# Two rows of TensorE products against one row interleaved by threes

## The chip, the cores and the metric

The kernel runs on one core of one Trainium2 chip. The metric is device time in microseconds (us), the median of several executions; lower is better.

## The reference

A linear attention layer feeds a dense two-layer network, and that feeds eight experts, of which each token takes one. All sizes are fixed: 2 x 768 = 1536 tokens, model width 384, dense width 2048, expert width 1024.

```
# attention: B, H, S, D = 2, 8, 768, 48
cur = k_t (outer) v_t * u ;  y_t = r_t @ (state + cur) ;  state = w * state + k_t (outer) v_t
# dense network on the 1536 x 384 result (the part that the change touches)
h = x @ w_in                                   # 384 -> 2048: "first layer"
g = np.where(h > 0.0, h, np.exp(np.minimum(h, 0.0)) - 1.0)
x2 = g @ w_out                                 # 2048 -> 384: "second layer"
# experts: argmax of x2 @ w_gate picks one of 8, at most 384 tokens each
h = np.maximum(np.einsum('ecd,edf->ecf', disp, w1), 0.0)
y = np.einsum('ecf,efd->ecd', h, w2)           # scaled by the gate and put back in token order
```

## The kernel before

Every float32 product is made of three faster products on values split in a high and a low half (`hi`, `lo`): hi x hi, hi x lo, lo x hi. The helper `product` issues these three matmuls, and so their lines in the profile are always L1362, L1363 and L1364, whatever they compute; the tile names tell them apart. `bank<-xt,wd_hi` with 256 moving columns is the first layer of the dense network, `bank<-wd_hi,g_hi` (or `g_lo`) with 392 moving columns the second (384 columns of x2 and 8 router logits).

The dense network runs over NB = 6 blocks n of 256 tokens, and in each over FT = 16 steps f of 128 hidden units; q = 16 n + f numbers the steps. In step q TensorE (PE) issues, in program order:

- `fc1(n, f)`: nine matmuls of the first layer (three slices of the model width, three matmuls each) into PSUM bank `ps_h[f % 2]`. The last one raises the semaphore `s_h`. Before the first, PE waits for `s_g` >= q - 1, that is, until the bank has been read for step q - 2.
- in some steps products of the attention (`scores`, `back`, `outer`), of the routing (`count`, `logits`) or transposes;
- `fc2` of three steps earlier (LAG = 3): six matmuls, three for each of the two tiles of 128 tokens, into `ps_x2[0]` and `ps_x2[1]`. Before the first, PE waits for `s_glo` of step q - 3. Sixteen such steps accumulate into one pair of banks. The last of a block (in step f = 2 of the next block) raises `s_fc2`; the first of the next block (in step f = LAG = 3) waits until both banks have been copied out (`s_x2`).

Between the two layers lies the function g, on four engines in a row for each step: VectorE (DVE) takes the minimum with 0 (L1182, which waits for `s_h`), ScalarE (ACT) the exponential (L866), VectorE the maximum (L1190, raises `s_g`), ScalarE rounds to the high half (L875, `s_ghi`), GpSimd (POOL) subtracts to get the low half (L707, `s_glo`). `elu` has two buffers, `g_hi` and `g_lo` have four. Each of these engines works its own list in order, and other work is written into that list behind the step's own part:

- VectorE: copying x2 out of its bank (L1155, in step f = 2 after L1190), and the router: `shift`, `choose`, `gates` and `place_rows` in steps 7, 8, 9 and 11 of block 1, in steps 3, 6, 7 and 9 of blocks 2 to 4, and in steps 3, 5, 6 and 9 of block 5; in block 5, from step 5 on, also the low halves of the first expert's weights (L1165), between L1182 and L1190.
- ScalarE: the other copy of x2 (L834), and in block 5 in every second step a cast of the first expert's weights (L856).
- GpSimd: keys, queries, decay and diagonals of the attention, and the scatter of routed rows (L683).

The order is written by hand; nothing is scheduled by a planner. A table (`PLANS`, read by `chunk_for`) says in which step a piece of the attention is due. `route(n)` is the same for the router.

Of the kernel before, what the change touches and what calls it, by code (L numbers as in the profile page):

```python
# [12 lines left out]
def build(nc, B, H, S, D, DFF, NE, FE, CAP, rkt_in, nat_in, decay, bonus, bonus_pair, win, wout, wouttr, wgate, wexp, out, slots):  # L13
    T = B * S
    C = 128
# [4 lines left out]
    KT = DM // 128  # L20
    BT = 2
    BN = BT * C
    NB = T // BN
    FT = DFF // 128
# [15 lines left out]
    LAG = 3  # L40
# [38 lines left out]
    def new(name, shape, dtype=F32):  # L79
        return put(name, shape, dtype)[0]  # L80
# [32 lines left out]
    wd_hi = new("wd_hi", [128, WI + FT * WO], F32R)  # L113
    wd_at = top[0]
    wd_lo = new("wd_lo", [128, WI + FT * WO], F32R)
# [8 lines left out]
    xt = [new(f"xt{b}", [128, KT, 2, BN], F32R) for b in range(2)]  # L124
    pwk2 = put("pwk2", [128, HP, C], F32, top[0])[0]
    g_hi = new("g_hi", [128, 4, BN], F32R)
    prod = put("prod", [128, 2, HP, C], F32, top[0])[0]
    g_lo = new("g_lo", [128, 4, BN], F32R)
# [48 lines left out]
    with ctx:  # L177
        bank = [ctx.enter_context(nc.psum_tensor(f"bank{i}", [128, 512], F32)) for i in range(8)]

        ps_h, ps_x2, ps_s, ps_y = bank[0:2], bank[2:4], bank[4:6], bank[6:8]  # L180
# [7 lines left out]
        def sem(name):  # L188
            return ctx.enter_context(nc.semaphore(name))
# [54 lines left out]
        s_h = sem("h_done")  # L244
        s_m = sem("min_ready")
        s_exp = sem("exp_ready")
        s_g = sem("g_ready")
        s_ghi = sem("g_hi_ready")
        s_glo = sem("g_lo_ready")
        s_fc2 = sem("fc2_done")  # L250
# [65 lines left out]
        F_T, F_LG = 3, 6  # L316
        F_WG, F_WGT = 12, 14

        def route(n):

            return dict(zip(("shift", "choose", "gates", "count", "place", "scatter"),
                            (7, 8, 9, 10, 11, 11) if n == 0 else
                            (3, 6, 7, 8, 9, 12) if n < NB - 2 else (3, 5, 6, 8, 9, 10)))
        F_W1 = 2
        F_X = 5
        F_A, F_E0 = 9, 5
# [33 lines left out]
        def chunk_for(what, n, f):  # L360

            for c, steps in PLANS.items():
                if steps.get(what) == FT * n + f:
                    return c
            return None
# [21 lines left out]
        def leaves_state(c):  # L387
            return c % PER != PER - 1
# [13 lines left out]
        def wait_if(eng, s, count):  # L402

            if not (isinstance(count, int) and count <= 0):
                eng.wait_ge(s, count)
# [4 lines left out]
        def w_in_cols(f, kt):  # L410

            return slice((f * KT + kt) * 128, (f * KT + kt + 1) * 128)
# [5 lines left out]
        def gated_cols(f):  # L418

            return slice(WI + f * WO, WI + (f + 1) * WO)  # L420

        def x2_cols(n):

            return slice(NE if n == 0 else 0, WO)
# [932 lines left out]
        def _(pe):  # L1357
            mm = nc.tensor.matmul

            def product(dst, w_hi, w_lo, x_hi, x_lo, start, stop):  # L1360

                mm(dst, w_hi, x_hi, start=start, stop=False)  # L1362
                mm(dst, w_hi, x_lo, start=False, stop=False)  # L1363
                return mm(dst, w_lo, x_hi, start=False, stop=stop)  # L1364
# [91 lines left out]
            def bonus_sums(c):  # L1456
                pe.wait_ge(s_up, 16)
                pe.wait_ge(s_prod, c + 1)
                for hp in range(HP):
                    last = mm(bonus_bank(c)[:, hp, :, :], rk_pair(c)[:, hp, :], bc(u_pair[:, hp, :].unsqueeze(1), [128, C // 4, 2]),  # L1460
                              start=True, stop=True)
                last.then_inc(s_bmm, 1)
# [7 lines left out]
            for hp in range(HP):  # L1470
                last = nc.tensor.transpose(ps_y[1][:, 128 * hp:128 * hp + 128], pwk2[:, hp, :], ident[:, :])
# [9 lines left out]
            def fc1(n, f):  # L1481
                q = FT * n + f
                wait_if(pe, s_g, q - 1)
                if n == 0:
                    pe.wait_ge(s_wlo, f + 1)
                x = xt[n % 2]
                if n == 0 and f == 0:
                    pe.wait_ge(s_xhi, 4)
                    for w in (wd_hi, wd_lo):
                        for kt in range(KT):  # L1490
                            mm(ps_h[0][:, 0:BN], w[:, w_in_cols(0, kt)], x[:, kt, 0, :], start=w is wd_hi and kt == 0,
                               stop=False)
                    pe.wait_ge(s_xlo, 4)
                    for kt in range(KT):
                        last = mm(ps_h[0][:, 0:BN], wd_hi[:, w_in_cols(0, kt)], x[:, kt, 1, :], start=False,
                                  stop=kt == KT - 1)
                    last.then_inc(s_h, 1)
                    return
                if f == 0:
                    pe.wait_ge(s_xlo, 4 * (n + 1))  # L1500
                for kt in range(KT):
                    cols = w_in_cols(f, kt)
                    last = product(ps_h[f % 2][:, 0:BN], wd_hi[:, cols], wd_lo[:, cols], x[:, kt, 0, :], x[:, kt, 1, :],
                                   kt == 0, kt == KT - 1)
                last.then_inc(s_h, 1)

            def fc2(n, f):
# [15 lines left out]
                if f == FT - 1:  # L1523
                    last.then_inc(s_fc2, 1)

            def early_x():
                pe.wait_ge(s_xr[0], 16)
                for kt in range(KT):
                    last = nc.tensor.transpose(ps_s[0][:, 128 * kt:128 * kt + 128],
                                               xrow[0][:, 0, 128 * kt:128 * kt + 128], ident[:, :])  # L1530
                last.then_inc(s_axtr, 1)
# [11 lines left out]
            def gated_transpose():  # L1543
                pe.wait_ge(s_wgt, 1)
                for i in range(4):
                    last = nc.tensor.transpose(ps_s[1][:, 128 * i:128 * i + 128], wg_tr[:, 128 * i:128 * i + 128],
                                               ident[:, :])
                last.then_inc(s_wgb, 1)
# [9 lines left out]
            def logits():  # L1558

                pe.wait_ge(s_gw, 16)  # L1560
                pe.wait_ge(s_xlo, 8)
                for t in range(BT):
                    pe.wait_ge(s_x2t[t], 1)
                for t in range(BT):
                    for kt in range(KT):
                        last = mm(ps_lg[:, NE * t:NE * (t + 1)], x2t[:, t, 128 * kt:128 * kt + 128],
                                  gate_w[:, kt, 0:NE], start=kt == 0, stop=kt == KT - 1)
                last.then_inc(s_lg, 1)
# [12 lines left out]

            for n in range(NB):
                for f in range(FT):
                    fc1(n, f)
                    if n == 1 and f == F_LG:
                        logits()
                    c = chunk_for("scores", n, f)
                    if c is not None:
                        scores(c)
                    if c == 2:  # L1590
                        bonus_sums(2)
                    c = chunk_for("back", n, f)
                    if c is not None:
                        back(c)
                    c = chunk_for("outer", n, f)
                    if c is not None and leaves_state(c):
                        outer(c)
                    if n == 0 and f == F_WG:
                        gated_w_out()
                    if n == 0 and f == F_WGT:  # L1600
                        gated_transpose()
                    if n == 1 and f == F_T:
                        for t in range(BT):
                            x2_transpose(t)
                    if n and f == route(n - 1)["count"]:
                        count(n - 1)
                    if n == NB - 1 and f == F_A:
                        early_x()
                    if f >= LAG:
                        fc2(n, f - LAG)  # L1610
                    elif n:
                        fc2(n - 1, FT + f - LAG)
# [58 lines left out]
            for f in range(ET):  # L1671
                if f % (ET // 2) == 0:
                    pe.wait_ge(s_aglo, 1 + 2 * f // ET)
                last = tile_fc2(f)
# [83 lines left out]
            for f in range(ET):  # L1758
                if f % (ET // 2) == 0:
                    pe.wait_ge(s_gelo, ET // 2 + f)  # L1760
                last = tile_fc2(f)
# [9 lines left out]
            with pe.If(over > SN):  # L1771
                with pe.Fori(0, NOVER) as e:
                    pe.wait_ge(s_dld, 32 * (e + 1))
                    for kt in range(KT):
                        last = nc.tensor.transpose(ps_xt[0][:, 128 * kt:128 * kt + 128],
                                                   xrow[0][:, 0, 128 * kt:128 * kt + 128], ident[:, :])
# [3 lines left out]
                    for f in range(ET):  # L1780
                        for kt in range(KT):
                            cols = slice(kt * FE + f * 128, kt * FE + (f + 1) * 128)
                            last = product(ps_e[f % 2][:, 0:128], we_hi[:, cols], we_lo[:, cols],
                                           xe_hi[0][:, kt, 0:128], xe_lo[0][:, kt, 0:128], kt == 0, kt == KT - 1)
                        last.then_inc(s_dh, 1)
                        pe.wait_ge(s_dgl, ET * e + f + 1)
                        cols = slice(W1 + f * DM, W1 + (f + 1) * DM)
                        last = product(ps_ye[0][:, 0:DM], ge_hi[:, f % 4, 0:128], ge_lo[:, f % 4, 0:128],
                                       we_hi[:, cols], we_lo[:, cols], f == 0, f == ET - 1)
# [80 lines left out]
```

## Time and profile before

| | |
|---|---|
| median of 3 executions | 415.98 us (415.86 to 416.11) |
| span of the profiled execution | 413.8 us |
| around the span (median less span) | 2.2 us |
| PE busy, share of the span | 98% |
| DVE / ACT / POOL busy | 59% / 45% / 56% |
| instructions in the profile | 9451 |

The time of a run is 2.2 us over the span between the first and the last instruction of the profiled execution. A busy TensorE is counted from a start to a modelled end, and consecutive matmuls overlap in the records, so the distance from start to start says what a matmul costs. The dense network takes the stretch from about 17 us to 264 us, the experts the rest.

### The profile page before, as it was taken

The page shows a single profiled execution, that of the slowest core. Times are in us where ns is not written, and L with a number is a line of the kernel's source. Part 1 is how long each engine was busy: PE and PEld are TensorE (multiplying, and loading weights), DVE is VectorE, ACT ScalarE, POOL GpSimd, SP SyncE. Part 2 cuts the span into 40 slices and gives each one's busy share as a digit, 9 for nine tenths or more (in the row PEclk, how much of TensorE's full clock was granted, in tenths as well). Part 3 has the DMA queues.
Part 4 walks back from the last instruction along what each step waited for, and adds up shares of the span by engine and source line. Part 5 has one row for each costly group of instructions (what it writes and reads, how often), then busy time and mean ns, then how long its engine had stood idle before and what let it go on. Part 6 is the DMA issues. An engine that isn't in the chain of part 4 may idle for free.

```text
span 413.8 us, 9451 instructions
## 1 busy us (share of the span) xinstructions
PE 406.2 (98%) x3697; PEld 390.8 (94%) x3697; DVE 243.7 (59%) x576; ACT 188.1 (45%) x409; POOL 231.0 (56%) x239
## 2 busy tenths in 40 slices
PE   8999999999999999999999999999999999999994
PEld 8799799999999999999999999999999999999994
DVE  7787955376576547654653487785635556364521
ACT  4786543233433333333343555553645445464420
POOL 3789775467856685668234336075073461825531
PEclk9999999999999999999999999999999999999999
DMA  7998996204030403020018001827383845729000
GB/s 287 402 396 351 367 344 243 82 38 148 12 119 2 139 21 118 3 86 21 2 20 344 2 2 38 326 77 248 125 308 101 340 160 203 295 89 360 5 31 28
DMA packets 18650, 64.98 MB, mean 157 GB/s; under 512 B 2203, under 2 KB 11717, under 8 KB 16432
## 3 DMA queue, kind: packets, MB, share of 16 engines
q1 hardware_dynamic: 16672, 59.67, 39.5%
q0 software_dynamic: 1792, 4.73, 3.0%
q8 instruction: 28, 0.46, 0.4%
q14 instruction: 14, 0.11, 0.1%
q10 hardware_dynamic: 144, 0.00, 0.0%
HBM read 51.98 MB, written 13.21 MB: 158 GB/s over the span
## 4 chain that ended last, share of the span: by engine, by line
PE 92%; DVE 4%; issue 1%; POOL 1%; ACT 1%; DMA 0%; POOLq 0%; DVEq 0%
PE bank L1362 27%; PE bank L1364 26%; PE bank L1363 26%; PE bank L1383 2%; PE bank L1412 1%; PE bank L1448 1%; PE bank L1452 1%; PE bank L1686 1%; PE bank L1441 1%; PE bank L1444 1%; PE bank L1539 1%; PE bank L1721 1%; PE bank L1722 1%; PE bank L1725 1%; PE bank L1625 1%
## 5 line engine op out<-in xcount | busy, mean ns | idle before, releaser
L707 POOL TENSOR_TENSOR g_lo<-elu,g_hi 128x256 fp32r<-128x256 f32 x95 | 73.8, 778 | 86.5 <-ACT g_hi L875 86.3
L1362 PE MATMUL bank<-xt,wd_hi 128*128 128x256 f32 x285 | 80.7, 283 | 0.6 <-DVE elu L1190 0.6
L1364 PE MATMUL bank<-xt,wd_lo 128*128 128x256 f32 x285 | 80.5, 282 | 0.0
L1363 PE MATMUL bank<-xt,wd_hi 128*128 128x256 f32 x285 | 80.4, 282 | 0.0
L866 ACT ACTIVATE elu<-elu 128x256 f32<-128x256 f32 x96 | 40.1, 418 | 76.5 <-DVE elu L1182 75.9
L1362 PE MATMUL bank<-wd_hi,g_hi 128*128 128x392 f32 (+1 forms) x192 | 67.5, 352 | 0.0
L1364 PE MATMUL bank<-wd_hi,g_lo 128*128 128x392 f32 (+1 forms) x192 | 65.3, 340 | 0.0
L1363 PE MATMUL bank<-wd_lo,g_hi 128*128 128x392 f32 (+1 forms) x192 | 65.2, 339 | 0.0
L1190 DVE SCALAR_TENSOR_TENSOR elu<-elu,bank 128x256 f32<-128x256 f32 x96 | 40.3, 420 | 40.5 <-ACT elu L866 40.5
L875 ACT CAST g_hi<-elu 128x256 fp32r<-128x256 f32 x96 | 39.0, 406 | 45.0 <-DVE elu L1190 45.0
L1362 PEld LDWEIGHTS bank<-xt,wd_hi 128*128 128x128 f32 x285 | 54.0, 189 | 1.3 <-DVE elu L1190 1.1
L1364 PEld LDWEIGHTS bank<-xt,wd_lo 128*128 128x128 f32 x285 | 54.2, 190 | 0.0
L1363 PEld LDWEIGHTS bank<-xt,wd_hi 128*128 128x128 f32 x285 | 54.1, 190 | 0.0
L1294 DVE SCALAR_TENSOR_TENSOR ge_lo<-bank,ge_hi 128x256 fp32r<-128x256 f32 x56 | 23.8, 425 | 48.8 <-ACT ge_hi L933 48.8
L1182 DVE TENSOR_SCALAR elu<-bank 128x256 f32<-128x256 f32 x80 | 33.8, 423 | 31.1 <-PE bank L1364 26.5
L933 ACT ACTIVATE ge_hi<-bank 128x256 fp32r<-128x256 f32 x56 | 21.6, 385 | 53.1 <-PE bank L1364 31.1
L724 POOL TENSOR_TENSOR wd_lo<-wd_raw,wd_hi 128x1024 fp32r<-128x1024 f32 x12 | 30.4, 2556 | 26.7 <-ACT wd_hi L946 24.3
L1362 PEld LDWEIGHTS bank<-wd_hi,g_hi 128*128 128x128 f32 x192 | 36.4, 189 | 2.0 <-issue 1.4
L1363 PEld LDWEIGHTS bank<-wd_lo,g_hi 128*128 128x128 f32 x192 | 36.4, 190 | 0.0
L724 POOL TENSOR_TENSOR we_lo<-we_raw,we_hi 128x1024 fp32r<-128x1024 f32 x9 | 21.3, 2398 | 26.9 <-ACT we_hi L946 26.9
L1364 PEld LDWEIGHTS bank<-wd_hi,g_lo 128*128 128x128 f32 x192 | 36.1, 188 | 0.0
L729 POOL DMA_INDIRECT out<-yrow,tok_i x16 | 15.7, 983 | 18.5 <-DVE yrow L1314 11.7
(220 smaller groups left out, 946.2 us busy)
## 6 DMA issues: line engine op xcount, KB each, us to landing
we_raw<-wexp SPq DMA_DIRECT2D x8, 1536.0 KB, 6.5
wd_raw<-wexp SPq DMA_DIRECT2D x8, 1536.0 KB, 7.7
rkt<-rkt SPq DMA_DIRECT2D x12, 512.0 KB, 5.5
nat<-nat SPq DMA_DIRECT2D x9, 672.0 KB, 5.0
xrow<-slots SPq DMA_DIRECT2D x16, 193.0 KB, 7.3
wd_raw<-win SPq DMA_DIRECT2D x4, 768.0 KB, 8.0
wd_raw<-wout SPq DMA_DIRECT2D x4, 768.0 KB, 8.9
wo_tr<-wouttr SPq DMA_DIRECT2D x1, 3072.0 KB, 17.8
```

Source lines behind the costliest of these rows:

```text
L707: nc.gpsimd.tensor_tensor(g_lo[:, f % 4, :], elu[:, f % 2, :], g_hi[:, f % 4, :].bitcast(F32), ALU.subtract).then_inc(s_glo, 1)
L724: nc.gpsimd.tensor_tensor(EL[r][:, cols], ER[r][:, cols], EH[r][:, cols].bitcast(F32), ALU.subtract).then_inc(s_elo2[r], 1)
L729: nc.gpsimd.indirect_dma_start(out=out, out_offset=bass.IndirectOffsetOnAxis(ap=tok_i[r][:, t, :], axis=0), in_=yrow[r][:, t, :], in_offse ...
L866: nc.scalar.activation(elu[:, f % 2, :], elu[:, f % 2, :], ACT.Exp, scale=-1.0 if n == 0 else 1.0).then_inc(s_exp, 1)
L875: nc.scalar.copy(g_hi[:, f % 4, :], elu[:, f % 2, :]).then_inc(s_ghi, 1)
L933: nc.scalar.activation(ge_hi[:, f % 4, :], ps_e[f % 2][:, 0:SN], ACT.Relu).then_inc(s_gehi, 1)
L1182: V.tensor_scalar_min(elu[:, f % 2, :], ps_h[f % 2][:, 0:BN], 0.0).then_inc(s_m, 1)
L1190: V.scalar_tensor_tensor(out=elu[:, f % 2, :], in0=elu[:, f % 2, :], scalar=-1.0, in1=ps_h[f % 2][:, 0:BN], op0=ALU.add, op1=ALU.max).then ...
L1294: V.scalar_tensor_tensor(out=ge_lo[:, f % 4, :], in0=ps_e[f % 2][:, 0:SN], scalar=0.0, in1=ge_hi[:, f % 4, :].bitcast(F32), op0=ALU.max, o ...
L1362: mm(dst, w_hi, x_hi, start=start, stop=False)
L1363: mm(dst, w_hi, x_lo, start=False, stop=False)
L1364: return mm(dst, w_lo, x_hi, start=False, stop=stop)
```

## The change

Two functions come in. `alone(n, f)` names the steps that hold nothing on TensorE but the two layers: it leaves out all of block 0, the first three steps of block 1, steps f = 0 and f = 3 of every block, and every step with attention, routing or transposed products. That leaves 53 of the 96 steps: 8 in block 1 (4, 5, 7, 8, 11, 12, 14, 15), 11 each in blocks 2 to 4 (1, 2, 4, 5, 6, 7, 10, 12, 13, 14, 15) and 12 in block 5 (the same and 11). In these `both` issues the step's fifteen matmuls as first layer x 3, second layer x 3 (tile 0), first x 3, second x 3 (tile 1), first x 3. The products, their operands, their number and the values waited for are the same; the wait for `s_glo` now stands behind three matmuls of the first layer.

```diff
+            def both(n, f, m, e):
+
+                q = FT * n + f
+                pe.wait_ge(s_g, q - 1)
+                x = xt[n % 2]
+                for kt in range(KT):
+                    cols = w_in_cols(f, kt)
+                    last = product(ps_h[f % 2][:, 0:BN], wd_hi[:, cols], wd_lo[:, cols], x[:, kt, 0, :], x[:, kt, 1, :],
+                                   kt == 0, kt == KT - 1)
+                    if kt == KT - 1:
+                        last.then_inc(s_h, 1)
+                        break
+                    if kt == 0:
+                        pe.wait_ge(s_glo, FT * m + e + 1)
+                    g = slice(kt * C, (kt + 1) * C)
+                    last = product(ps_x2[kt][:, x2_cols(m)], g_hi[:, e % 4, g], g_lo[:, e % 4, g], wd_hi[:, gated_cols(e)],
+                                   wd_lo[:, gated_cols(e)], False, e == FT - 1)
+                    if kt == BT - 1 and e == FT - 1:
+                        last.then_inc(s_fc2, 1)
+
+            def alone(n, f):
+
+                if n == 0 or f == 0 or f == LAG or (n == 1 and f < LAG):
+                    return False
+                if any(chunk_for(what, n, f) is not None for what in ("scores", "back", "outer")):
+                    return False
+                return f not in (route(n - 1)["count"], F_A) and not (n == 1 and f in (F_T, F_LG))
+
...
             for n in range(NB):
                 for f in range(FT):
+                    if alone(n, f):
+                        both(n, f, n if f >= LAG else n - 1, (f - LAG) % FT)
+                        continue
                     fc1(n, f)
```

On TensorE, before, step (5, 2) and the beginning of step (5, 3) stand like this (names in brackets are the semaphores waited for: `g_ready` is `s_g`, `g_lo_ready` is `s_glo`, `x2_ready0` and `x2_ready1` are the copies out of the two x2 banks):

```order
1484 L1362 MATMUL bank<-xt_84,wd_hi 128x256
1485 L1363 MATMUL bank<-xt_84,wd_hi 128x256
1486 L1364 MATMUL bank<-xt_84,wd_lo 128x256
1487 L1362 MATMUL bank<-wd_hi,g_hi 128x392 [waits g_lo_ready]
1488 L1363 MATMUL bank<-wd_lo,g_hi 128x392
1489 L1364 MATMUL bank<-wd_hi,g_lo 128x392
1490 L1362 MATMUL bank<-wd_hi,g_hi 128x392
1491 L1363 MATMUL bank<-wd_lo,g_hi 128x392
1492 L1364 MATMUL bank<-wd_hi,g_lo 128x392
1493 L1362 MATMUL bank<-xt_84,wd_hi 128x256 [waits g_ready]
```

Row 1486 is the ninth matmul of the first layer, which raises `s_h`; six of the second layer follow it. After the change the same engine has, at the same place:

```order
1478 L1362 MATMUL bank<-xt_84,wd_hi 128x256 [waits g_ready]
1479 L1363 MATMUL bank<-xt_84,wd_hi 128x256
1480 L1364 MATMUL bank<-xt_84,wd_lo 128x256
1481 L1362 MATMUL bank<-wd_hi,g_hi 128x392 [waits g_lo_ready]
1482 L1363 MATMUL bank<-wd_lo,g_hi 128x392
1483 L1364 MATMUL bank<-wd_hi,g_lo 128x392
...
1490 L1362 MATMUL bank<-xt_84,wd_hi 128x256
1491 L1363 MATMUL bank<-xt_84,wd_hi 128x256
1492 L1364 MATMUL bank<-xt_84,wd_lo 128x256
1493 L1362 MATMUL bank<-xt_84,wd_hi 128x256 [waits g_ready]
```

The wait for `g_lo_ready` moved up from row 1487 to row 1481, and the matmul that raises `s_h` moved down from row 1486 to row 1492, the last before the next step.

## Rows read from the trace of the kernel before

**Rows 1.** The page: busy time of TensorE, and the chain that ended last.

```profile
PE 406.2 (98%) x3697; PEld 390.8 (94%) x3697; DVE 243.7 (59%) x576; ACT 188.1 (45%) x409; POOL 231.0 (56%) x239
...
PE 92%; DVE 4%; issue 1%; POOL 1%; ACT 1%; DMA 0%; POOLq 0%; DVEq 0%
```

**Rows 2.** What TensorE waited for: total us, times, longest.

```profile
PE bank L1362 <- DVE elu L1190: 0.6, 2, 0.3
```

**Rows 3.** Timeline of steps (5, 2) and (5, 3): start, duration, engine, line.

```profile
229.39 0.28 PE L1362 MATMUL bank<-xt,wd_hi 128*128 128x256 f32 x1
...
230.35 0.28 PE L1364 MATMUL bank<-xt,wd_lo 128*128 128x256 f32 x1
230.35 0.19 PEld L1362 LDWEIGHTS bank<-wd_hi,g_hi 128*128 128x128 f32 x1
...
230.47 0.35 PE L1362 MATMUL bank<-wd_hi,g_hi 128*128 128x392 f32 x1
230.47 0.19 PEld L1363 LDWEIGHTS bank<-wd_lo,g_hi 128*128 128x128 f32 x1
230.65 0.34 PE L1363 MATMUL bank<-wd_lo,g_hi 128*128 128x392 f32 x1
...
230.67 0.42 DVE L1182 TENSOR_SCALAR elu<-bank 128x256 f32<-128x256 f32 x1 [0.83 <-PE bank L1364]
...
231.13 0.42 ACT L866 ACTIVATE elu<-elu 128x256 f32<-128x256 f32 x1 [0.85 <-DVE elu L1182]
...
231.36 0.34 PE L1364 MATMUL bank<-wd_hi,g_lo 128*128 128x392 f32 x1
...
231.54 0.28 PE L1362 MATMUL bank<-xt,wd_hi 128*128 128x256 f32 x1
...
231.58 0.42 DVE L1190 SCALAR_TENSOR_TENSOR elu<-elu,bank 128x256 f32<-128x256 f32 x1 [0.48 <-ACT elu L866]
...
231.91 0.56 DVE L1155 COPY x2row<-bank 128x392 f32<-128x392 f32 x1
...
232.62 0.41 PE L1362 MATMUL bank<-wd_hi,g_hi 128*128 128x392 f32 x1
...
232.88 0.34 PE L1363 MATMUL bank<-wd_lo,g_hi 128*128 128x392 f32 x1
```

**Rows 4.** Timeline of block 1: `s_g` of step (1, 9), start of step (1, 11).

```profile
89.00 0.42 DVE L1190 SCALAR_TENSOR_TENSOR elu<-elu,bank 128x256 f32<-128x256 f32 x1 [0.48 <-ACT elu L866]
...
89.48 0.39 PE L1362 MATMUL bank<-xt,wd_hi 128*128 128x256 f32 x1 [0.30 <-DVE elu L1190]
```

**Rows 5.** Timeline of blocks 2 and 3: `s_g` of step 7, start of step 9.

```profile
124.28 0.42 DVE L1190 SCALAR_TENSOR_TENSOR elu<-elu,bank 128x256 f32<-128x256 f32 x1 [0.48 <-ACT elu L866]
...
125.50 0.28 PE L1362 MATMUL bank<-xt,wd_hi 128*128 128x256 f32 x1
...
165.63 0.42 DVE L1190 SCALAR_TENSOR_TENSOR elu<-elu,bank 128x256 f32<-128x256 f32 x1 [0.48 <-ACT elu L866]
...
166.97 0.27 PE L1362 MATMUL bank<-xt,wd_hi 128*128 128x256 f32 x1
```

**Rows 6.** Timeline, GpSimd from (2, 12) and (3, 12) to 14; TensorE in (3, 1).

```profile
138.52 0.74 POOL L707 TENSOR_TENSOR g_lo<-elu,g_hi 128x256 fp32r<-128x256 f32 x1 [2.81 <-ACT g_hi L875]
...
145.27 0.75 POOL L707 TENSOR_TENSOR g_lo<-elu,g_hi 128x256 fp32r<-128x256 f32 x1
...
147.13 0.35 PE L1362 MATMUL bank<-wd_hi,g_hi 128*128 128x392 f32 x1
...
186.72 0.76 POOL L707 TENSOR_TENSOR g_lo<-elu,g_hi 128x256 fp32r<-128x256 f32 x1
```

**Rows 7.** Timeline of block 5: a weight cast, `s_g` of step 11, start of step 13.

```profile
251.27 1.05 ACT L856 CAST we_hi<-we_raw 128x1024 fp32r<-128x1024 f32 x1
...
252.99 0.41 DVE L1190 SCALAR_TENSOR_TENSOR elu<-elu,bank 128x256 f32<-128x256 f32 x1
...
253.59 0.28 PE L1362 MATMUL bank<-xt,wd_hi 128*128 128x256 f32 x1
```

## The prediction

> **What bounds the kernel now.** I read the page first: TensorE is busy for 98% of the span and makes up 92% of the chain that ended last [rows 1]. Then the waits of TensorE: in the whole program it waited for the function g between the layers only twice, 0.6 us together [rows 2]. So while the dense network runs, each us in which TensorE issues nothing is a us of the result, and the three other engines matter only where they make it wait. The question is then how much room they have, which the timeline of one step without other work shows [rows 3]. Read it so: the step begins with the first layer at 229.39, the second layer begins at 230.47, the next step at 231.54. That is 2.15 us a step, 1.08 for nine first-layer matmuls (0.12 each) and 1.07 for six second-layer matmuls (0.18 each). The ninth first-layer matmul ends at 230.35 + 0.28 = 230.63; VectorE starts 0.04 later (230.67), ScalarE follows (231.13), VectorE ends its second operation at 231.58 + 0.42 = 232.00. So g is ready 1.37 us after the first layer's end.
>
> The bank that this frees is wanted by the first layer two steps later, at 231.54 + 2.2 = about 233.7. The room is 1.7 us.
>
> **The change, part by part.** Nothing is added or removed. What moves is (a) the matmul that raises s_h, (b) the wait for g_lo, (c) the neighbours of each matmul.
>
> (c) Neighbours. From the last first-layer matmul to the first second-layer one the distance is 230.47 - 230.35 = 0.12, the distance within the first layer; at the other seam it is 231.54 - 231.36 = 0.18, that of the second layer [rows 3]. A seam costs nothing that the rows can show. The change adds two seams to each of 53 steps, 106 in all. The rows are rounded to 0.01, so the bounds are -0.5 and +0.5 us; I take 0, which is what both seams read.
>
> (a) The signal. In the 53 steps the ninth first-layer matmul is now the last of fifteen. It starts 0.12 before the next step, ends at 231.54 - 0.12 + 0.28 = 231.70, not 230.63: **1.07 us later**. All that hangs on it comes 1.07 later, while the first layer two steps on does not move. The room in a plain step falls from 1.7 to 0.6 us: still enough, so no wait in most of the 53. Below 1.07 us before, there is one now. I looked for each such place.
>
> 1. Block 1. Step (1, 8) holds choose, (1, 9) gates. VectorE is already behind there: its L1190 of step 9 ends at 89.00 + 0.42 = 89.42, and TensorE starts step 11 at 89.48, having waited 0.30 for it [rows 4]. Steps 7 and 8 are both interleaved, so VectorE's whole list from there shifts by 1.07, and its backlog hands this on to step 9. There is no room: **1.07**.
>
> 2. Blocks 2 and 3, choose in step 6, gates in step 7. L1190 of step 7 ends at 124.28 + 0.42 = 124.70, step 9 starts at 125.50. With 1.07 more and the 0.06 that TensorE needs after the signal (89.42 to 89.48) it can start at 125.83: 0.33 late. In block 3: 165.63 + 0.42 + 1.13 = 167.18 against 166.97, 0.21 late [rows 5]. A matmul that starts from a wait costs a little more: 232.62 to 232.88 is 0.26 where 0.18 is usual [rows 3], so 0.08 each. **0.41 and 0.29**. In block 4 VectorE is less behind; I take 0.
>
> 3. The copy of x2 in block 5. The first second-layer matmul of step (5, 3), at 232.62, needs both x2 banks copied. VectorE's copy ends at 231.91 + 0.56 = 232.47, 0.15 before it: this wait is met almost exactly today [rows 3]. The last second-layer matmul of step 2 comes some 0.36 us earlier after the change, but VectorE's list has L1190 of step 2 ahead of the copy, and that is 1.07 late. So the copy ends at 233.54. **1.07**, with its slow start already in the 0.26. In blocks 2 to 4 the attention's products stand between the two layers in step 3 and cover it; were they gone, it would be 1.07 in each.
>
> (b) The wait for g_lo. It moves ahead of six first-layer matmuls, 0.71 us, and g_lo comes up to 1.07 later: 1.78 us less room.
>
> 4. GpSimd in steps 12 to 14 of blocks 2 and 3 works without a pause from the g_lo of step 12 (138.52, for which it had waited) through keys, two scatters, decay and queries to that of step 14, which ends at 145.27 + 0.75 = 146.02. TensorE wants it at 147.13, in step (3, 1). After: ready 146.02 + 1.07 + 0.06 = 147.15, wanted 147.13 - 0.71 = 146.42. 0.73 late, with the slow start 0.81. The same run ends at 187.48 in the next block (41.46 later, the same place in step (4, 1)) [rows 6]. **1.62** for the two. In block 4 no keys are left to make, and the run is shorter.
>
> 5. The end of block 5. From step 5 on VectorE and ScalarE also split the first expert's weights; a cast takes 1.05 (251.27) and sits between two steps of g. The tightest place is step 11: L1190 ends at 252.99 + 0.41 = 253.40, step 13 starts at 253.59. After: 254.53, 0.94 late, with the slow start **1.02** [rows 7]. The choose and gates of this block lie on the way and are part of this sum, since the lateness is handed on. Item 3 delays both sides by the same time, and is added.
>
> Sum: 1.07 + 0.41 + 0.29 + 1.07 + 1.62 + 1.02 = 5.5 us. After block 5 nothing is caught up, for TensorE is the chain [rows 1]. Against the profiled execution the span becomes 413.8 + 5.5 = 419.3 us; the median of the runs shown is 2.2 above the span, 415.98 + 5.5 = **421.5 us**, +1.3%.
>
> What could it gain? Two things come earlier: g_lo is read 0.7 us sooner, and the x2 banks are full 0.36 us sooner. No row shows TensorE waiting for either, so I count nothing.
>
> **The rivals.** 0.2% (0.8 us) is about what a measurement can tell from no change.
>
> A. The forecast. With item 1 and both 1.07s certain and the rest half as large it is 3.8 us; with each seam 0.01 worse and half as much again on items 2, 4 and 5 it is 8.2. Own range 419.0 to 424.3. Chance 0.80.
>
> B. Slower by less: VectorE's or GpSimd's lateness is not handed on. For it: a step leaves VectorE idle 0.83 before L1182, and 0.46 to 0.48 inside [rows 3], in which a backlog melts. Against: where the list is full, as in item 4, there are no gaps. If only items 1 and 3 stay, 2.1 us: 418.1. Chance 0.08.
>
> C. No difference: also items 1 and 3 find room. Point of decision: the 0.15 us before the copy and the 0.06 in block 1 would have to be 1.07. Time 416.0. Chance 0.03.
>
> D. Faster. A weight load starts with the product ahead of its own (230.35 for the one at 230.47, 230.47 for the one at 230.65), one product ahead and no more [rows 3]. If it could run further ahead, the longer second-layer matmuls would make room for loads, and the first-layer ones behind them might start closer than 0.12. If each of 53 x 9 gained 0.013, it would be 6.2 us, which beats the 5.5 of stalls: 415.3; the point of decision is 0.0115 a matmul. Against it: the loads are in step with the products on both sides of both seams. Chance 0.03. The Trainium skill, "TensorE: Matmul & The Clock Gate", section "Back-to-back issue gap", has the spacing "set by both ops, pipelined through the 64-deep reorder window", which would favour such mixing; by its isolated gap N / 2.4 + 2.5 ns a first-layer product could come every 109 ns (an estimate from that page), 11 ns under the row's, worth 5.2 us over 53 steps. No row here shows a load more than one product ahead.
>
> E. Worse. The room of 0.6 us in plain steps is not there, because three first-layer triples each meet a late bank or engine. If g took 0.7 us more than 1.37 in every step, 40 plain steps would lose 0.1 each on top: 425.5. The rows show 1.37 to 0.01 us in quiet steps, so I give it 0.06.
>
> **How the numbers follow.** The predicted time is A's. 418.5 to 424.5 holds nearly all of A, the upper half of B, and leaves out C, D and E and the rest of B. Slower by over 0.2%: A, B, E, 0.94, less 0.01 for a B that shrinks under 0.8 us, 0.93. Same: C with that, 0.04. Faster: D, 0.03.
>
> **What the profile after would show.** TensorE's waits for elu L1190 go from 0.6 to about 3 us, and waits for x2row L1155 (about 1) and g_lo L707 (about 1.5) are new, at the five places and hardly elsewhere. L1182 starts at the beginning of a step, not in its middle. Plain steps keep 2.15 us. If they become 2.05, D is right. If TensorE shows waits in plain steps, E. If the waits are there and the time is not, what is wrong is that TensorE is the chain. The likeliest mistake is in the sizes of items 4 and 5, where several engines hand a delay on.

## The result and the profile after

The changed kernel takes 421.22 us (median of 4 executions, 420.99 to 421.90) against 415.92 us for the kernel before on the same chip: a ratio of 1.0137, 95% interval 1.0125 to 1.0149 (the two medians alone give 1.0127). By the medians that is 5.3 us more. The profiled execution took 420.99 us, its span is 419.1 us against 413.8.

From the page after, the row of busy times and the chain that ended last, which answer to [rows 1]:

```profile
PE 408.2 (97%) x3697; PEld 390.7 (93%) x3697; DVE 241.1 (58%) x576; ACT 188.1 (45%) x409; POOL 231.9 (55%) x239
...
PE 74%; DVE 8%; issue 6%; POOL 6%; DMA 3%; ACT 3%; POOLq 0%; SPq 0%; DVEq 0%
```

The engines' work is the same to 1% or so and TensorE still looks full. The chain tells more: TensorE's part of it fell from 92% to 74%, because the chain now leaves TensorE at each wait, and follows VectorE, ScalarE and GpSimd back. The waits of TensorE name the places (engine, line <- releaser: total us, times, longest), and answer to [rows 2]:

```profile
PE bank L1362 <- DVE elu L1190: 1.3, 3, 0.8
PE bank L1466 <- DVE x2t L986: 1.1, 1, 1.1
PE bank L1362 <- POOL g_lo L707: 1.1, 2, 0.6
PE bank L1362 <- DVE x2row L1155: 0.9, 1, 0.9
PE bank L1441 <- DVE att L1031: 0.3, 1, 0.3
PE bank L1606 <- DVE n_seen L1124: 0.3, 1, 0.3
```

L1466 is the start of the program and is as it was. Two waits for g_lo, one for the copy of x2 and one for `n_seen` are new. These sums are less than what is lost, since idle time is counted from the modelled end of the matmul before; so the wait for g shows as 1.3 us, where the prediction wanted to see about 3. What is lost is better read from the starts of the steps. These are step starts in the timeline of TensorE after the change:

```profile
90.05 0.39 PE L1362 MATMUL bank<-xt,wd_hi 128*128 128x256 f32 x1 [0.77 <-DVE elu L1190]
...
126.34 0.38 PE L1362 MATMUL bank<-xt,wd_hi 128*128 128x256 f32 x1
...
150.00 0.28 PE L1362 MATMUL bank<-xt,wd_hi 128*128 128x256 f32 x1
...
169.26 0.27 PE L1362 MATMUL bank<-xt,wd_hi 128*128 128x256 f32 x1
...
192.76 0.28 PE L1362 MATMUL bank<-xt,wd_hi 128*128 128x256 f32 x1
...
230.31 0.27 PE L1362 MATMUL bank<-xt,wd_hi 128*128 128x256 f32 x1
...
237.88 0.28 PE L1362 MATMUL bank<-xt,wd_hi 128*128 128x256 f32 x1
...
246.78 0.39 PE L1362 MATMUL bank<-xt,wd_hi 128*128 128x256 f32 x1 [0.22 <-DVE elu L1190]
...
258.59 0.39 PE L1362 MATMUL bank<-xt,wd_hi 128*128 128x256 f32 x1
```

They are steps (1, 11), (2, 9), (3, 2), (3, 9), (4, 2), (5, 1), (5, 4), (5, 8) and (5, 13). The lag behind the same step of the kernel before (its start subtracted) grows at a few places only, and stands still to 0.03 us everywhere else:

| place | lag after it, us | growth there | term of the prediction |
|---|---|---|---|
| (1, 11), g of (1, 9) | 0.58 | 0.47 | 1.07 |
| (2, 9) and (2, 10), `count` in step (2, 8), then g | 0.94 | 0.31 + 0.10 | 0.41 |
| (3, 1) to (3, 2), g_lo of (2, 14) | 1.77 | 0.81 | 0.81 |
| (3, 9), `count` in step (3, 8) | 2.29 | 0.52 | 0.29 |
| (4, 1) to (4, 2), g_lo | 3.09 | 0.80 | 0.81 |
| (5, 3) to (5, 4), copy of x2 | 4.12 | 1.07 | 1.07 |
| (5, 8) to (5, 14), g at (5, 8), (5, 9), (5, 12), (5, 13) | 5.09 | 1.01 | 1.02 |
| end of the span | 5.30 | 0.21 | - |

Before (1, 11) the lag was already 0.1; it was there at the first step of the dense network, before any interleaved one.

The row of (3, 9) needs a closer look. `count` in step (3, 8) starts with `n_seen`, the second layer follows. Before and after the change:

```profile
165.57 0.17 PE L1578 MATMUL bank<-n_seen,ones_r 128*128 128x8 f32 x1
...
165.82 0.43 PE L1362 MATMUL bank<-wd_hi,g_hi 128*128 128x392 f32 x1
```

```profile
167.78 0.24 PE L1606 MATMUL bank<-n_seen,ones_r 128*128 128x8 f32 x1 [0.28 <-DVE n_seen L1124]
...
168.11 0.43 PE L1362 MATMUL bank<-wd_hi,g_hi 128*128 128x392 f32 x1
```

With the lag of 1.77 `count` was due at 167.34; it starts 0.44 later. The second layer is then at 168.11 - 165.82 = 2.29, the whole lag of (3, 9): at (3, 9) itself TensorE does not wait for g. In block 2 `count` holds the second layer of (2, 8) up by 0.28 in the same way (124.35 before, 125.16 after, with a lag of 0.53), and g, which is ready just behind it, sets the start of (2, 9).

The longest plain stretch is the best proof for the price of a seam. From (4, 2) to (5, 1) the changed kernel takes 230.31 - 192.76 = 37.55 us; the kernel before starts these steps at 189.68 and 227.24, 37.56 us. Ten of the steps between are interleaved, with 20 seams more, and cost nothing.

The place of the copy of x2, from the timeline after, steps (5, 2) and (5, 3), answers to [rows 3]:

```profile
234.59 0.28 PE L1362 MATMUL bank<-xt,wd_hi 128*128 128x256 f32 x1
...
234.78 0.42 DVE L1182 TENSOR_SCALAR elu<-bank 128x256 f32<-128x256 f32 x1 [0.82 <-PE bank L1364]
...
235.69 0.42 DVE L1190 SCALAR_TENSOR_TENSOR elu<-elu,bank 128x256 f32<-128x256 f32 x1 [0.48 <-ACT elu L866]
236.03 0.56 DVE L1155 COPY x2row<-bank 128x392 f32<-128x392 f32 x1
...
236.74 0.42 PE L1362 MATMUL bank<-wd_hi,g_hi 128*128 128x392 f32 x1 [0.91 <-DVE x2row L1155]
...
236.99 0.34 PE L1363 MATMUL bank<-wd_lo,g_hi 128*128 128x392 f32 x1
```

Step (5, 3) starts at 234.59; L1182 of step (5, 2) starts 0.19 after that, where it used to start 0.87 before it (230.67 against 231.54). The copy ends at 236.59, and the second layer starts 0.15 later: 2.15 us after the start of the step, where it was 1.08.

### The profile page after: what moved, and what is told of

Same layout as the page of the kernel before. It is cut to its first block, busy times and chain, and to the rows that moved or that the text cites. A ratio compares the mean times of both kernels' runs of the same rounds, so it can differ in the third digit from the quotient of the medians.

```text
span 419.1 us, 9451 instructions
## 1 busy us (share of the span) xinstructions
PE 408.2 (97%) x3697; PEld 390.7 (93%) x3697; DVE 241.1 (58%) x576; ACT 188.1 (45%) x409; POOL 231.9 (55%) x239
## 4 chain that ended last, share of the span: by engine, by line
PE 74%; DVE 8%; issue 6%; POOL 6%; DMA 3%; ACT 3%; POOLq 0%; SPq 0%; DVEq 0%
PE bank L1362 22%; PE bank L1364 20%; PE bank L1363 20%; DMA xrow<-slots 2%; POOL g_lo L707 2%; PE bank L1383 2%; DVE elu L1190 1%; DVE elu L1182 1%; ACT elu L866 1%; PE bank L1717 1%; ACT we_hi L856 1%; PE bank L1412 1%; DVE we_lo L1165 1%; PE bank L1448 1%; PE bank L1452 1%
## 5 line engine op out<-in xcount | busy, mean ns | idle before, releaser
L707 POOL TENSOR_TENSOR g_lo<-elu,g_hi 128x256 fp32r<-128x256 f32 x95 | 74.1, 781 | 91.0 <-ACT g_hi L875 90.6
L1182 DVE TENSOR_SCALAR elu<-bank 128x256 f32<-128x256 f32 x80 | 33.7, 422 | 42.2 <-PE bank L1364 36.5
```

What stands on the lines that cost most here:

```text
L707: nc.gpsimd.tensor_tensor(g_lo[:, f % 4, :], elu[:, f % 2, :], g_hi[:, f % 4, :].bitcast(F32), ALU.subtract).then_inc(s_glo, 1)
L1182: V.tensor_scalar_min(elu[:, f % 2, :], ps_h[f % 2][:, 0:BN], 0.0).then_inc(s_m, 1)
```

## The experiments

Each kernel was compared with the kernel before on the same chip. Only the order of the work was changed in them. The chips differ a little (the kernel before has medians of 415.74 to 416.00), so two kernels are compared here by what each is over before; the change is 5.3 over. Medians of four or five executions that lie 1 us apart fix such a difference to half a microsecond or so, and the sizes of single waits come from the traces. The letters of rivals in the expectations are those of each experiment, not those of the prediction.

**1. Keep the interleaving only where I saw room.** One more line in `alone`:

```diff
+                if n == NB - 1 or (n, f) in ((1, 7), (1, 8), (3, 1), (4, 1)) or (n in (2, 3, 4) and f in (6, 7, 12)):
+                    return False
```

> The interleaving is kept in 28 of the 53 steps only, those whose late signal I find room for: none in block 5, none in steps (1, 7), (1, 8), (3, 1), (4, 1), none in steps 6, 7 and 12 of blocks 2 to 4. Theory A (time is lost only where an engine's list is full and hands on the 1.07 us): within 0.4 us of before, about 416.0, TensorE's waits as before. Rival B (the order itself costs, 5.3 us / 53 = 0.10 us a step): 28 x 0.10 = 2.8 us slower than before, 418.7.

Measured: 416.58 us, before 416.00; ratio 1.0016 (1.0007 to 1.0025), 0.6 us more, not 2.8. Rival B falls. But 0.6 is above my 0.4, and in its interval (0.3 to 1.0). In the trace the lag is at most 0.02 up to (1, 13), grows by 0.39 in the attention products of that step, by 0.13 + 0.10 at (2, 9) and (2, 10) and by 0.35 at (3, 9), and by 0.00 in the interleaved steps between. So two of my "quiet" places were not: step (n, 5) is interleaved there and its late g starts `choose` in step 6 late. The 0.39 is something else: the four traces of this chip (this run and the next three) have it, 0.37 to 0.39 where it can be read, whatever the order of the steps, and the nine other traces have not, that of the change among them, though run 3 has the same instructions there. Nothing shows that the change causes it. Without it the trace gives 0.23 + 0.35 = 0.58, which is what was measured.

**2. As late a signal without interleaving.** The loop in `both` was written anew over a list of triples, `('h', k)` for three first-layer matmuls and `('x2', k)` for three of the second layer, with the waits and signals as they were (s_g before the first `h`, s_glo before the first `x2`, s_h with the last `h`). Here the order is second layer x 6, then first layer x 9:

```diff
-                for kt in range(KT):
+                for what, k in [('x2', 0), ('x2', 1), ('h', 0), ('h', 1), ('h', 2)]:
```

> In the 53 steps the six second-layer matmuls come first and the nine first-layer ones behind them, as two rows: no seam more than before, but the signal is as late as in the change (1.07 us). Theory A: the wait for the copy of x2 stays (1.07), the two waits for g_lo grow from 0.8 to about 1.15 each, since it is now wanted another 0.36 us earlier; the first layer starts 1.07 later too, so waits for g stay only where the step two on is not of the 53 (blocks 2, 3 and 5, steps 8 and 9, about 1.3 in all), and go in (1, 11) and (5, 13). Sum about 4.7 us over before: 420.7. Rival B (the seams cost): as before, 416.

Measured: 422.31 us, before 416.00; ratio 1.0153 (1.0140 to 1.0167), 6.3 us more. Two whole rows cost more than the threes do, so the cost is that of the place of the signal and of the wait, and not of the mixing. TensorE's waits in this run:

```profile
PE bank L1362 <- POOL g_lo L707: 1.8, 2, 0.9
...
PE bank L1362 <- DVE x2row L1155: 0.9, 1, 0.9
PE bank L1362 <- DVE elu L1190: 0.9, 3, 0.4
```

The waits for g_lo grew from 1.1 to 1.8 us, 0.35 each for a wait that stands 0.36 us earlier: as expected. The lag at (3, 3) and (4, 3) grew by 1.17 each. My sum of 4.7 was 1.6 too low. It left out block 1, where the lag grew by 0.7 up to (1, 13), and the 0.55 us in (1, 13), part of which is the 0.39 of above.

**3. Without step (5, 2)**, which stays as two rows:

```diff
+                if (n, f) == (NB - 1, LAG - 1):
+                    return False
```

> The change without step (5, 2), which stays as two rows. Theory A: exactly the wait for the copy of x2 goes, 1.07 us of the 5.3: 420.1, 4.2 us over before. Rival B: one step in 53, 0.1 us: 421.1.

Measured: 420.17 us, before 416.00; ratio 1.0105 (1.0090 to 1.0121), 4.2 us more, as expected. One step of 53 carries 1.1 of the 5.3 us, and rival B's 0.1 falls. TensorE's wait for x2row is gone from the list of waits, but not all of the loss: the lag still grows by 0.16 at (5, 4), against 1.07. Step (5, 1) is interleaved too and its late g puts VectorE's copy back to 235.44 to 236.00, 0.15 before the second layer of (5, 3) at 236.15. By the trace the step is worth 0.9.

**4. The copy of x2 ahead of g**, step (5, 2) stays interleaved:

```diff
+                    if n == NB - 1 and f == LAG - 1:
+                        x2_rows(n - 1)
                     act.wait_ge(s_m, q + 1)
...
+                    if n == NB - 1 and f == LAG - 1:
+                        x2_rows(n - 1)
                     if n:
                         dve.wait_ge(s_h, q + 1)
```

(and the later call left out for that block on both engines.)

> The change with all 53 steps, but in step (5, 2) VectorE and ScalarE copy x2 out before their own part of g, not behind it. Theory A: the wait in step (5, 3) goes though the products stay interleaved, 1.07 us less, 420.1. Rival C (the wait hangs on the second-layer products themselves, not on VectorE's order): no change, 421.2.

Measured: 420.51 us, before 416.00; ratio 1.0113 (1.0096 to 1.0130), 4.5 us more. That is 0.8 less than the change, with an interval (4.0 to 5.4 over before) that holds both the expected 4.2 and the 5.3; the time alone does not decide. The trace does: at (5, 4) the lag changes by -0.07, where it was +1.07. It shows both copies at the earlier place, beside the interleaved products:

```profile
234.76 0.49 ACT L834 COPY x2row<-bank 128x392 f32<-128x392 f32 x1
234.76 0.57 DVE L1157 COPY x2row<-bank 128x392 f32<-128x392 f32 x1 [0.46 <-PE bank L1368]
```

The second layer of (5, 3) starts at 236.00, 0.12 after the matmul before it, without a wait. Rival C falls: the wait hung on VectorE's list.

**5 and 6. How late the signal, how early the wait.** Both kernels signal 0.53 us late. Run 5 (first line) waits for g_lo where the change does, run 6 (second line) 0.36 us later:

```diff
+                for what, k in [('h', 0), ('x2', 0), ('h', 1), ('h', 2), ('x2', 1)]:
...
+                for what, k in [('h', 0), ('h', 1), ('x2', 0), ('h', 2), ('x2', 1)]:
```

> Order in the 53 steps: first x 3, second x 3, first x 6, second x 3. As many seams as in the change and g_lo waited for at the same place, but the first layer's signal is only 0.53 us later than before, not 1.07. Theory A: copy of x2 0.53, g_lo twice about 0.27, block 5 about 0.45, block 1 up to 0.2, blocks 2 and 3 nothing: 1.8 us over before, 417.7. Rival B (the seams cost): 421.2.

Measured: 417.68 us, before 415.75; ratio 1.0045 (1.0032 to 1.0059), 1.9 us more.

> Order: first x 6, second x 3, first x 3, second x 3. The signal 0.53 us later than before as in the run with first x 6 in the middle, but g_lo is waited for only 0.36 us earlier than before, not 0.71. Theory A: the same without the two waits for g_lo, 1.25 us over before, 417.2; no wait of TensorE for g_lo. Rival B (the seams cost): 421.2.

Measured: 416.61 us, before 415.75; ratio 1.0022 (1.0013 to 1.0031), 0.9 us more. The traces: at (3, 2) and (4, 2) the lag of run 5 grows by 0.33 and 0.34, that of run 6 not at all. At (5, 4) both grow by 0.53, exactly the lateness of the signal. So with one order of 15 matmuls the two causes come apart: halving the lateness of the signal took more than half of the loss, for the room of 0.6 us is used up only by what is above it (in blocks 2 and 3 the lag does not grow at step 9). Both orders have the same number of seams as the change, so seams cannot cost more than the 0.9 us of run 6 in all. My "up to 0.2" for block 1 was wrong: at (1, 11) both traces lose 0.53 and 0.54, the whole lateness. Run 6 measured less than my 1.25 even so; its traced execution (417.39) is the slowest of eleven, and shows 1.8 us over before where the median is 0.9 over.

**7 and 8. The two ends of GpSimd's run.** Run 7 is without (3, 1) and (4, 1), where g_lo is waited for, run 8 without (2, 12) and (3, 12), where the run of GpSimd begins:

```diff
+                if (n, f) in ((3, 1), (4, 1)):
+                    return False
...
+                if (n, f) in ((2, 12), (3, 12)):
+                    return False
```

> The change without steps (3, 1) and (4, 1), which stay as two rows. Theory A: the two waits for g_lo go (ready at 147.15 against 147.13 wanted, by the rows of before), 1.6 us less: 419.6, 3.7 over before. Rival B: 0.2 us less, 421.0.

Measured: 420.47 us, before 415.75; ratio 1.0109 (1.0093 to 1.0124). Of the 1.6 us only 0.6 went (4.7 over before), by the trace 0.7 at these two places. In the trace the wait for g_lo is gone, but another stands behind it (TensorE, VectorE and GpSimd around step (3, 2)):

```profile
147.35 1.44 POOL L707 TENSOR_TENSOR g_lo<-elu,g_hi 128x256 fp32r<-128x256 f32 x2
...
148.21 0.42 DVE L1182 TENSOR_SCALAR elu<-bank 128x256 f32<-128x256 f32 x1 [1.73 <-POOL g_lo L707]
...
149.11 0.42 DVE L1190 SCALAR_TENSOR_TENSOR elu<-elu,bank 128x256 f32<-128x256 f32 x1 [0.48 <-ACT elu L866]
...
149.59 0.19 PEld L1362 LDWEIGHTS bank<-xt,wd_hi 128*128 128x128 f32 x1 [0.42 <-DVE elu L1190]
149.59 0.39 PE L1362 MATMUL bank<-xt,wd_hi 128*128 128x256 f32 x1
```

L1182 of step (3, 0) writes the `elu` buffer that GpSimd still reads for g_lo of (2, 14). It waited 1.73 us for it, g of (3, 0) is late in turn, and the first layer of (3, 2) starts 0.35 us late, with 0.11 more behind it. I had not looked for this path.

> The change without steps (2, 12) and (3, 12), where GpSimd's unbroken run begins; steps (3, 1) and (4, 1), where TensorE waited for g_lo, stay interleaved. Theory A with two paths (a late g_lo stops TensorE directly in (3, 1), and by way of VectorE, whose L1182 of (3, 0) waits for that g_lo, in (3, 2)): both paths go, twice 0.8 us less than the change, 419.6, while leaving out (3, 1) and (4, 1) took only twice 0.35. Rival E (only the earlier reading of g_lo counts): 0.2 us less.

Measured: 419.38 us, before 415.74; ratio 1.0085 (1.0071 to 1.0098), 3.6 over before and so 1.7 less than the change. Both paths are gone: the lag does not grow at (3, 2) or (4, 2), though (3, 1) and (4, 1) are interleaved and wait for g_lo as early as in the change. The cause is the lateness with which GpSimd's run starts; rival E falls.

**9. Without (1, 7) and (1, 8).**

```diff
+                if (n, f) in ((1, 7), (1, 8)):
+                    return False
```

> The change without steps (1, 7) and (1, 8). The prediction counted 1.07 us for block 1, the trace of the change shows 0.47 at the start of step (1, 11). Theory A: 0.5 us less than the change, 420.7. If the 1.07 is there and hidden elsewhere: 420.1. Rival B: 0.2 us less, 421.0.

Measured: 420.34 us, before 415.75; ratio 1.0109 (1.0094 to 1.0125), 4.6 over before and so 0.7 less than the change. In this trace the lag at (1, 11) is 0, and the other places are as in the change. 0.7 is between my 0.5 and 1.1 and cannot tell them apart; rival B's 0.2 does not fit the trace. The next runs say why both sizes can occur.

**10 and 11. What VectorE waits for in block 1.** Small operations of `shift` and `choose` are odd there. VectorE and GpSimd before the change:

```profile
86.30 0.74 DVE L1122 TENSOR_TENSOR before<-before,onehot 128x8 fp32r<-128x8 f32 x1
87.08 1.11 DVE L1124 TENSOR_TENSOR n_seen<-before,onehot 128x8 fp32r<-128x8 f32 x1
```

```profile
86.29 0.73 POOL L707 TENSOR_TENSOR g_lo<-elu,g_hi 128x256 fp32r<-128x256 f32 x1 [1.05 <-ACT g_hi L875]
86.98 1.18 POOL L648 TENSOR_TENSOR r<-rkt,powers 128x512 f32<-128x512 f32 x1
```

L1122 ends at 87.04 and GpSimd's operation at 87.02; L1124 ends at 88.19 and GpSimd's next at 88.16. In the kernel before and in the change I moved that next one, L648 (queries of chunk 6), from step (1, 8) to (1, 9):

```diff
             if c == 6:
-                steps.update(rk=b - 4, with_u=b - 3)
+                steps.update(rk=b - 4, with_u=b - 3, queries=b - 4)
```

> The kernel before, with one GpSimd multiply (queries of chunk 6, 1.2 us) moved from step (1, 8) to step (1, 9). Theory A2 (small VectorE operations on 128 x 8 values in block 1 end only when the GpSimd operation beside them ends: L1122 and L1124 take 0.74 and 1.11 us instead of 0.17): L1124 shrinks from 1.11 to about 0.17, VectorE is about 0.9 us less behind, TensorE's wait of 0.30 at step (1, 11) and its small follower go: 0.5 us faster than before, 415.4. Rival D (these durations are the operations' own): no change, L1124 stays at 1.11.

Measured: 415.09 us, before 415.74; ratio 0.9986 (0.9977 to 0.9995), 0.6 us **faster than the kernel before**, the only kernel here that is. L1124 in this run:

```profile
87.29 0.17 DVE L1124 TENSOR_TENSOR n_seen<-before,onehot 128x8 fp32r<-128x8 f32 x1
```

1.11 became 0.17. The wait of 0.30 at the start of (1, 11) [rows 4] is gone: of TensorE's two waits for g [rows 2] one is left, and step (1, 11) starts 0.47 us earlier against the kernel before, (1, 12) another 0.11. Rival D falls.

> The change, with the same multiply moved from (1, 8) to (1, 9). Theory A2: the 0.47 us of block 1 in the change and the 0.3 to 0.5 that the kernel before loses there go, about 0.9 us less than the change: 420.3. Rival D: no change, 421.2.

Measured: 420.23 us, before 415.74; ratio 1.0103 (1.0088 to 1.0118), 4.5 over before and so 0.8 less than the change, where 0.9 was expected; L1124 takes 0.17 us here too.

With this the 1.07 and the 0.47 can be told apart. The profiles of the change and of run 8 have the same instructions up to block 2. In the change L1104 (a cast of 128 x 8 values in `shift`) starts at 84.53, 0.02 behind GpSimd's L707, and takes 0.15:

```profile
84.51 0.78 POOL L707 TENSOR_TENSOR g_lo<-elu,g_hi 128x256 fp32r<-128x256 f32 x1 [5.40 <-ACT g_hi L875]
...
84.53 0.15 DVE L1104 CAST before<-n_seen 128x8 fp32r<-128x8 f32 x1
```

In run 8 it starts at 84.50, also 0.02 behind it, and takes 0.74, as in the kernel before:

```profile
84.48 0.74 POOL L707 TENSOR_TENSOR g_lo<-elu,g_hi 128x256 fp32r<-128x256 f32 x1 [5.41 <-ACT g_hi L875]
...
84.50 0.74 DVE L1104 CAST before<-n_seen 128x8 fp32r<-128x8 f32 x1
```

There the lag grows by 0.25 + 0.82 = 1.07 at (1, 10) and (1, 11), the size of the prediction. With the same instructions up to there, the traces of the change and of runs 3, 4 and 7 show 0.15 to 0.16, and that of run 8 alone 0.74. In both cases the cast starts 0.02 us behind L707; what decides between them is not shown, but it is worth 0.6 us of the result.

## Why the prediction was right

- **What bounds.** TensorE's room was the right measure: each us that it started late is in the result. The lag never shrinks again by more than 0.03 us from one step to the next.
- **(c) Neighbours, 0 us.** Shown: 20 seams in 37.55 us cost -0.01; and two whole rows (run 2) cost more than the threes. The prediction's rival D needed 0.0115 us a first-layer matmul; no load of the two layers starts more than one product ahead in the trace after either, and plain steps take 2.13 to 2.15 us.
- **Item 3, 1.07 us: measured 1.07** in the trace. Leaving the step out gave back 1.1 by the medians and 0.9 by the trace, moving the copy 1.14 by the trace.
- **Item 4, 1.62 us: measured 0.81 + 0.80**, caused by the late start of GpSimd's run (run 8). The mechanism was incomplete: a second path by way of the `elu` buffer hid behind the first and kept 0.46 us of each when the first was taken away (run 7).
- **Item 5, 1.02 us: measured 1.01** over (5, 8) to (5, 14). Half of it is lost before the place that the item names: 0.50 at (5, 8) and (5, 9), 0.40 at (5, 13) and (5, 14). No run takes this item apart from item 3, so its cause is read from the trace only.
- **Item 2: 0.41 was 0.41 in block 2, 0.29 was 0.52 in block 3.** The step that failed is that only the bank's release was looked at. `count` in step (3, 8) waits for `choose` of step 6, and in block 3 it started 0.44 us late for it, 0.52 with the slow start; the wait for g that the item names did not occur there. In block 2 both waits lie on top of each other (0.28 by `count`), and the 0.41 came out right since g is the later one.
- **Item 1, mis-sized: 1.07 was 0.47 in the profiled execution.** "VectorE's backlog hands this on" held for the operations, but 0.6 us of the backlog was itself a wait for GpSimd that one execution has and another has not.
- The sum came out at 5.5 against 5.3 us since the misses in item 1 (-0.60) and in item 2 (+0.23), the 0.1 at the start and the 0.2 at the end of the span partly cancel. That is luck. The 0.1 is not of the change: this start lies 0.01 to 0.30 us behind that of before in the other traces, that of run 10 among them, which has no interleaved step. The 0.2 comes at 390 us, in the experts, where transposes of rows that a DMA brings start late; in the trace of run 7 TensorE waits 0.28 us there for that DMA and 0.22 at another such place, and its lag grows by 0.9 behind the dense network. It comes and goes with the execution, and why is open.
- The prediction's rivals B, C and E: lateness was handed on at each item (in block 1 by 0.47 of 1.07 us), and plain steps showed no wait.

## What to carry to other kernels

Before moving an instruction that signals, list every wait on the engine that bounds, with its room: the end of the releaser against the start of the waiting row. A signal moved by x costs x minus the room at each place, and nothing at the others; the sum of such differences gave 5.5 us for 5.3, though most of the 53 steps cost nothing. When a wait is taken away, look for the next one with nearly the same lateness (here the `elu` buffer) before counting its whole size as a gain. A short operation that takes several times its usual time and ends with another engine's operation is a wait, and moving the other engine's operation can be worth more than reordering the bounding one.

## What the runs showed of the hardware

VectorE and GpSimd in step (3, 6) after the change, whose `choose` holds up `count` in step (3, 8):

```profile
165.57 0.96 DVE L1118 SCALAR_TENSOR_TENSOR key<-lg,rank 128x16 f32<-128x16 f32 x1
166.57 0.17 DVE L1120 TENSOR_REDUCE col<-key 128x2 f32<-128x16 f32 x1
166.77 0.46 DVE L1121 TENSOR_TENSOR onehot<-key,col 128x16 fp32r<-128x16 f32 x1
```

```profile
165.31 1.19 POOL L648 TENSOR_TENSOR r<-rkt,powers 128x512 f32<-128x512 f32 x1
166.47 0.73 POOL L707 TENSOR_TENSOR g_lo<-elu,g_hi 128x256 fp32r<-128x256 f32 x1
```

L1118 ends at 166.53, GpSimd's L648 at 166.50; L1121 ends at 167.23, L707 at 167.20; the reduction L1120 between them runs beside L707 and takes its usual 0.17. Small VectorE operations on SBUF (128 x 8 or 128 x 16 values, 0.15 to 0.22 us as a rule) took 0.46 to 1.11 us and ended within 0.04 us of a GpSimd operation that ran beside them; with that one moved, 1.11 became 0.17. L1118, L1121, L1122 and L1124, which read two SBUF tensors, and the cast L1104 did so; the reductions did not. The Trainium skill, "SBUF — State Buffer", section "Who interferes with whom", says that a VectorE instruction with two SBUF inputs contends with a GpSimd instruction that reads SBUF, that a cast can do so, that the loser waits for the whole instruction, and that reductions never do. The traces agree in all four (0.46 to 1.11 us against 0.17, the cast's 0.74, the common end, the reduction's 0.17). They add that a cast which starts 0.02 us behind the GpSimd operation can fall either way (0.15 or 0.74 us).

A matmul that starts from a wait costs 0.07 to 0.11 us beyond it: its follower starts 0.25 later (236.74 to 236.99 in step (5, 3)) where 0.18 is usual, and 0.23 later (90.05 to 90.28 in step (1, 11)) where 0.12 is. And matmuls with 256 and 392 moving columns, each with its own weights, cost 0.12 and 0.18 us whatever their neighbours are. Busy times by stretch, from (4, 2) to (5, 1), of the change and then of the kernel before (busy us of each engine, granted clock, DMA share):

```profile
192.70:230.31 37.61, 37.61 (x389) 36.30 (x389) 20.31 (x60) 13.85 (x37) 16.37 (x23) 1.00 0.26 101
```

```profile
189.60:227.24 37.64, 37.64 (x389) 36.34 (x388) 20.26 (x59) 13.93 (x37) 16.74 (x22) 1.00 0.27 101
```

The granted clock is 1.00, the 2.4 GHz level, in both, and also in every other stretch in which TensorE works; it is lower only in the last 4 us (0.62 after, 0.85 before), where TensorE has nothing to do. So no part of the difference is the clock's.
